# The opening of a fused attention and two-layer kernel: the first two pairs of heads stacked from PSUM instead of by DMA

## The chip, the cores and the metric

The kernel runs on one NeuronCore of a Trainium2 chip. The metric is device time in microseconds (us) of one execution. Engines are named as in the profile: PE is the TensorE matmul engine, DVE is VectorE, ACT is ScalarE, POOL is GpSimd, SP is SyncE (here it only issues DMAs).

## What is computed

```python
# q, k, v: (4, 8, 576, 64) float32; 32 heads in 16 pairs
scores = scale * np.matmul(q, k.transpose(0, 1, 3, 2)); causal mask
a = softmax(scores); local = np.matmul(a, v)
q_p = phi(q)                                  # elu(q) + 1
mem_out = (q_p @ M_prev) / (q_p @ z_prev + 1e-06)
attn = g * mem_out + (1 - g) * local          # g = sigmoid(beta), per head
x = attn as (2304, 512)
x = (s * relu(x @ w_in)**2 + b) @ w_out                # 512 -> 2048 -> 512
out = solu_layernorm(x @ w_in2) @ w_out2               # 512 -> 1024 -> 512
```

## The kernel before

The kernel is three stages one after the other: attention, a squared-relu layer, a second layer. The change touches only how attention begins. Every engine has its own program, written out by hand in order, and the engines meet at semaphores: `sem.wait_ge(n)` holds the whole queue of that engine until the semaphore has reached n. Nothing reorders instructions within an engine.

Attention works on pairs of heads (64 of the 128 partitions each). For each pair `p`:

- SP loads the keys and queries (`load_keys`, `load_queries`) as five tiles of 128 rows; PE turns them (`turn_keys`, `turn_queries`: five 128x128 transposes each) into PSUM.
- To multiply in split precision, each operand is a rounded part and a rest. ACT rounds the keys (`round_keys`) into `cut[p]`, copies the queries into `qT` (`copy_queries`) and once more into `Q1` (`repeat_queries`); POOL rounds the queries (`round_queries`) and takes the rest (`cut_queries`); DVE takes the rest of the keys into `K1` (`cut_keys`).
- The score matmul contracts over 128 partitions: the head's own 64 rows and a second block of 64 rows beside them, kept in `stacked`. Since one of the blocks has to be moved to the other half of the partitions, SP does it with four DMAs from `cut` to `stacked` (`stack(p)`).

For each head `h` PE then makes five tiles of row scores in three steps (`first_rows`, `second_rows`, `third_rows`), each of which waits for the step before to have been read by DVE. DVE takes the row maxima (`row_maximum`, two or more instructions for each step). `first_rows(h+1)` also turns the maxima of head h; DVE copies them (`negT`), POOL spreads them over `Q1` (`spread_maxima`). After that `cross(h, 0..3)` computes the transposed scores minus the maxima, ACT exponentiates them (`exp_weights`), POOL masks the diagonal tiles (`mask_weights`), and `weigh_values(h, ...)` multiplies by the values. `memory(p)` multiplies the features of the queries (`feature_relu`, `feature_exp` on ACT, `features` on POOL) by the memory; DVE scales its result (`scale_memory`).

In the regular steps PE has, in step h, the rows of head h+2, the cross scores of head h and the values of head h-1. The kernel before enters them at h = -6, where most of it is not there yet. The clearing of buffers (memsets) stands at the start of DVE and POOL, and POOL clears `K1` (`clear_keys`) in step -2.

## Time and profile before

| | us |
|---|---|
| median of 3 runs | 879.56 (879.08 to 879.67) |
| profiled execution, time | 879.05 |
| profiled execution, span | 877.3 |
| PE busy | 853.0 (97%) |
| DVE, ACT, POOL busy | 492.0, 312.6, 259.3 |

Time and span of the profiled execution differ by 1.75 us, which lie outside the instructions. PE is busy nearly all the time except in the opening: in the first two of the page's 40 slices it shows 3 and 8 tenths and 9 or more from the third slice to the last but one. A view of the timeline gives each instruction's start and length and, in brackets, how long its engine sat idle before it and what ended that. Busy times of POOL are rough, and the ends of matmuls are modelled.

### The profile page before, as it was taken

How to read it: one execution, taken by the hardware profiler on the slowest of the kernel's cores; microseconds unless marked ns; L12 is line 12 of the kernel's file. 1: busy time of each engine (PE TensorE's matmuls, PEld its weight loads, DVE VectorE, ACT ScalarE, POOL GpSimd, SP SyncE). 2: the span in 40 equal slices, each digit the busy share in tenths (PEclk: the TensorE clock that was granted, in tenths of full speed). 3: DMA queues.
4: the chain of work that ended last, by engine and by line, in shares of the span. 5: the costliest groups of instructions: out<-in, count | busy, mean ns of one | idle time of the engine just before them, and what ended most of it. 6: DMA issues, size and time to landing. Idle time of an engine off the chain costs nothing.

```text
span 877.3 us, 13230 instructions
## 1 busy us (share of the span) xinstructions
PE 853.0 (97%) x4896; PEld 752.0 (86%) x4896; DVE 492.0 (56%) x1025; ACT 312.6 (36%) x564; POOL 259.3 (30%) x369
## 2 busy tenths in 40 slices
PE   3899999999999999999999999999999999999998
PEld 2799999999988888888888889999998888888886
DVE  6566666666546865433443344344758556566664
ACT  3555655656442223222322222232134232223322
POOL 6356565656559994000000000000600000000000
PEclk8799999999999999999999999999999999999999
DMA  7967575756503332000000000000220000000000
GB/s 168 162 141 160 125 155 131 157 129 142 124 1 97 109 107 73 1 1 1 0 1 1 1 0 1 1 1 1 73 72 1 25 25 24 24 24 24 12 24 37
DMA packets 87511, 51.63 MB, mean 59 GB/s; under 512 B 65184, under 2 KB 73376, under 8 KB 87456
## 3 DMA queue, kind: packets, MB, share of 16 engines
q1 hardware_dynamic: 86112, 50.59, 24.1%
q8 instruction: 35, 0.57, 0.3%
q10 hardware_dynamic: 1344, 0.30, 0.2%
q14 instruction: 20, 0.16, 0.1%
HBM read 27.28 MB, written 4.72 MB: 36 GB/s over the span
## 4 chain that ended last, share of the span: by engine, by line
PE 87%; DVE 7%; issue 2%; DMA 1%; POOL 1%; ACT 1%; SPq 0%; ACTq 0%; DVEq 0%; POOLq 0%
PE ps_h L923 7%; PE ps_h L925 7%; PE ps_h L924 7%; PE ps_y L938 7%; PE ps_y L939 7%; PE ps_y L940 7%; PE ps_v L499 7%; PE ps_s L440 4%; PE ps_hid L1199 4%; PE ps_r L1228 4%; PE ps_hid L1201 4%; PE ps_r L1230 4%; PE ps_hid L1200 4%; PE ps_r L1229 4%; PE ps_t L394 2%
## 5 line engine op out<-in xcount | busy, mean ns | idle before, releaser
L1042 DVE TENSOR_TENSOR xT<-xT 128x512 f32<-128x512 f32 (+1 forms) x80 | 60.7, 759 | 134.0 <-ACT xT L998 133.9
L938 PE MATMUL ps_y<-g_hi,wout 128*128 128x512 f32 (+1 forms) x320 | 117.6, 367 | 0.2 <-DVE g_lo L1049 0.2
L923 PE MATMUL ps_h<-x_hi,win 128*128 128x512 f32 (+1 forms) x320 | 117.7, 368 | 0.0
L925 PE MATMUL ps_h<-x_hi,win 128*128 128x512 f32 (+1 forms) x320 | 117.5, 367 | 0.0
L940 PE MATMUL ps_y<-g_hi,wout 128*128 128x512 f32 (+1 forms) x320 | 117.5, 367 | 0.0
L939 PE MATMUL ps_y<-g_lo,wout 128*128 128x512 f32 (+1 forms) x320 | 117.5, 367 | 0.0
L924 PE MATMUL ps_h<-x_lo,win 128*128 128x512 f32 (+1 forms) x320 | 117.5, 367 | 0.0
L499 PE MATMUL ps_v<-v_raw,pT 128*128 128x65 f32 (+1 forms) x960 | 107.5, 254 | 1.2 <-DVE t_loc L740 1.2
L499 PEld LDWEIGHTS ps_v<-v_raw,pT 128*128 128x128 f32 (+1 forms) x960 | 101.2, 173 | 6.6 <-issue 4.5
L678 DVE CUSTOM_DVE_ANT_0 spent<-ps_s,mask 128x576 f32<-128x576 f32 (+4 forms) x160 | 81.6, 539 | 44.4 <-PE ps_s L440 43.7
L561 ACT ACTIVATE pT<-ps_x 128x512 f32<-128x512 f32 (+3 forms) x128 | 64.0, 500 | 99.6 <-PE ps_x L484 98.6
L998 ACT ACTIVATE xT<-ps_h 128x512 f32<-128x512 f32 (+1 forms) x80 | 44.2, 553 | 148.4 <-PE ps_h L925 146.5
L1004 ACT ACTIVATE g_hi<-xT 128x512 fp32r<-128x512 f32 (+1 forms) x80 | 47.2, 590 | 132.3 <-DVE xT L1044 132.3
L1049 DVE TENSOR_TENSOR g_lo<-xT,g_hi 128x512 fp32r<-128x512 f32 (+1 forms) x80 | 63.4, 793 | 51.9 <-ACT g_hi L1004 51.9
L904 POOL TENSOR_SCALAR win<-stage 128x1024 fp32r<-128x1024 f32 x4 | 4.9, 1226 | 280.8 <-PE ps_h L925 280.8
L1186 POOL TENSOR_TENSOR rstd<-variance,minus_half 128x1 f32<-128x1 f32 x18 | 16.8, 931 | 212.8 <-DVE variance L1405 212.8
L344 POOL TENSOR_SCALAR_AFFINE_SELECT pT<-pT 128x128 f32<-128x128 f32 (+1 forms) x160 | 42.4, 284 | 94.9 <-ACT pT L561 94.9
L440 PE MATMUL ps_s<-stacked 128*128 128x512 f32 (+2 forms) x192 | 58.5, 388 | 10.7 <-DMA stacked<-cut 6.2
L938 PEld LDWEIGHTS ps_y<-g_hi,wout 128*128 128x128 f32 x320 | 60.1, 188 | 8.0 <-DVE g_lo L1049 0.5
L925 PEld LDWEIGHTS ps_h<-x_hi,win 128*128 128x128 f32 x320 | 60.1, 188 | 7.6
L923 PEld LDWEIGHTS ps_h<-x_hi,win 128*128 128x128 f32 x320 | 60.1, 188 | 7.5
L924 PEld LDWEIGHTS ps_h<-x_lo,win 128*128 128x128 f32 x320 | 60.1, 188 | 7.5
(130 smaller groups left out, 1677.2 us busy)
## 6 DMA issues: line engine op xcount, KB each, us to landing
stacked<-cut SPq DMA_DIRECT2D x64, 288.0 KB, 5.2
out<-res SPq DMA_DIRECT2D x18, 256.0 KB, 2.0
k_raw<-in_k SPq DMA_DIRECT2D x32, 128.0 KB, 2.6
v_raw<-in_v SPq DMA_DIRECT2D x32, 128.0 KB, 2.7
stage<-in_moe_w_in SPq DMA_DIRECT2D x16, 256.0 KB, 2.7
stage<-in_moe_w_out SPq DMA_DIRECT2D x16, 256.0 KB, 2.6
q_raw<-in_q SPq DMA_DIRECT2D x30, 128.0 KB, 3.7
stage<-in_moe_w_in SPq DMA_DIRECT2D x4, 512.0 KB, 3.4
```

What stands on the lines that cost most here:

```text
L440: ins = pe.matmul(ps_s[:, S_AT[t] + lo:S_AT[t] + hi], stacked[:, a, 0, P * t:P * (t + 1)], stacked[:, a, 1, lo:hi], start=True, stop=True)
L499: ins = pe.matmul(ps_v[0:m, par, E1 * t:E1 * (t + 1)], pT[par][:, at:at + m], v_raw[h // 2 % 3][:, j, par, :], start=(t == 0), stop=(j == ...
L561: act.activation(pT[h % 2][:, chunk_at[c]:chunk_at[c] + chunk_width[c]], ps_x[:, c % 2, 0:chunk_width[c]], ACT.Exp, scale=SCALE).then_inc( ...
L678: return dve.tensor_tensor_reduce(spent[:, at:at + n], ps_s[:, S_AT[t]:S_AT[t] + n], mask[:, FULL * P + r - n:FULL * P + r], -1.0, HUGE, A ...
L923: pe.matmul(out, hi, x_hi[:, k, 0:n], start=(k == 0), stop=False)
L924: pe.matmul(out, hi, x_lo[:, k, 0:n], start=False, stop=False)
L925: ins = pe.matmul(out, lo, x_hi[:, k, 0:n], start=False, stop=(k == KT - 1))
L938: pe.matmul(out, wout[:, f, HI, w], g_hi[:, r, 0:n], start=(f == 0), stop=False)
L939: pe.matmul(out, wout[:, f, HI, w], g_lo[:, r, 0:n], start=False, stop=False)
L940: ins = pe.matmul(out, wout[:, f, LO, w], g_hi[:, r, 0:n], start=False, stop=(f == FT - 1))
L1042: dve.tensor_tensor(r, r, r, ALU.mult).then_inc(square_done, 1)
L1049: dve.tensor_tensor(g_lo[:, f % RING, 0:width(c)], r, g_hi[:, f % RING, 0:width(c)], ALU.subtract)\
```

## The change

The first two pairs (heads 0 to 3) no longer use the DMA to stack. Their tiles are loaded into places with room for three 64-wide blocks (`first_k`, `first_q`, laid over `pT` and `t_mem`); DVE copies the first head's block behind the second's (`double`), so that PE can turn each pair in both head orders (`turn_keys` and `turn_swapped_keys`, and the same for queries). Every block of `stacked` then already lies on the right partitions in PSUM, and ACT (14 instructions named in `BY_ACT`) and DVE (6, in `BY_DVE`) write it from there. POOL repeats head 0's and head 2's queries (`repeat_first`). Pairs from 2 on are stacked by DMA as before. The first two head steps are written out by hand on each engine, in another order; PE starts with ten 128x128 matmuls on the identity (`warm_up`) whose result nobody reads; `memory(1)` moves from step 1 to step 2; the clearing of `K1` on POOL and DVE moves to their opening memsets; the first loads no longer wait for memsets.

```diff
-    t_mem = [sb(f"t_mem{s}", [P, NT, 2, D]) for s in range(3)]
+    all_t_mem = sb("t_mem", [P, 3 * NT * 2 * D])
+    t_mem = [all_t_mem[:, s * NT * 2 * D:(s + 1) * NT * 2 * D].rearrange("p (t two d) -> p t two d", two=2, d=D)
+             for s in range(3)]
...
+    THREE = NT * 3 * D
+    first_k, first_q = ([words_.rearrange("p (t three d) -> p t three d", three=3, d=D) for words_ in places]
+                        for places in ((pT[0][:, 0:THREE], all_t_mem[:, 0:THREE]),
+                                       (pT[1][:, 0:THREE], all_t_mem[:, THREE:2 * THREE])))
...
+    DIRECT = 2
+    BY_ACT = [(0, "k_own0"), (0, "k_moved0"), (0, "q_hi0"), (0, "q_cut0"), (0, "q_hi1"), (0, "q_own1"),
+              (1, "k_moved0"), (1, "k_moved1"), (1, "k_own0"), (1, "q_hi0"), (1, "q_cut0"), (1, "q_hi1"),
+              (1, "k_own1"), (1, "q_own1")]
+    BY_DVE = [(0, "k_own1"), (0, "k_moved1"), (0, "q_lo0"), (0, "q_lo1"), (1, "q_lo0"), (1, "q_lo1")]
+    K_SWAPPED, Q_SWAPPED = (1, 3), (2, 4)
...
+    DVE_CLEARS = PSUM_CLEARS + 3 + 2 * 2
+    WARM = 10
...
-        sp.wait_ge(cleared_dve, 1)
         load_keys(0)
-        sp.wait_ge(cleared_dve, 2)
-        load_queries(0)
-        sp.wait_ge(cleared_dve, 3)
         load_keys(1)
         load_keys(2)
         load_queries(2)
-        stack(0)
-        stack(1)
-        load_keys(3)
         load_memory()
         load_values(0)
+        load_keys(3)
         load_queries(3)
         load_values(1)
-        for h in range(HEADS):
+        stack(2)
+        load_keys(4)
+        for h in range(1, HEADS):
...
-        def clear_keys():
-            pool.memset(words(K1[:, :, :, S:W]), 0.0).then_inc(cleared, 1)
-            pool.memset(words(K1[MINE[0], :, 1, 0:S]), 1.0).then_inc(cleared, 1)
-            pool.wait_ge(cleared, POOL_CLEARS)
+        pool.memset(words(K1[:, :, :, S:W]), 0.0).then_inc(cleared, 1)
+        pool.memset(words(K1[MINE[0], :, 1, 0:S]), 1.0).then_inc(cleared, 1)
+        pool.wait_ge(cleared, POOL_CLEARS)
+        def repeat_first(p):
+            act_placed(pool, p, "q_hi0")
+            pool.tensor_scalar(Q1[MINE[0], p, 0, 0:S], words(stacked[MINE[0], slot(2 * p), 0, 0:S]), 1.0, 1.0,
+                               ALU.mult, ALU.mult).then_inc(repeated, 1)
...
+        repeat_first(0)
+        repeat_first(1)
+        pool.wait_ge(repeated, DIRECT)
+        spread_maxima(0)
+        mask_weights(0, 0)
+        round_queries(2)
+        mask_weights(0, 1)
+        cut_queries(2)
+        features(0)
+        mask_weights(0, 3)
+        features(1)
+        pool.wait_ge(phi_done, 2)
+        spread_maxima(1)
+        mask_weights(1, 0)
+        mask_weights(1, 1)
+        pool.wait_ge(tri_done, NT + 4)
+        spread_maxima(2)
+        mask_weights(1, 3)
...
+        def turn_swapped(raw, into):
+            for t in range(NT):
+                ins = pe.transpose(into[:, P * t:P * (t + 1)],
+                                   raw[:, t, 1:3, :].rearrange("p two d -> p (two d)"), ident[:, :])
+            ins.then_inc(swapped_turned, 1)
+        def warm_up():
+            for _ in range(WARM):
+                pe.matmul(ps_s[:, 0:P], ident[:, :], ident[:, :], start=True, stop=True)
...
+            elif p == 1:
+                act_placed(pe, 0, "k_own0")
+                pe.wait_ge(k_lo_done, 1)
...
+            if h < 2 * DIRECT:
                 p = h // 2
-                pe.wait_ge(stack_landed[p % SLOTS][h % 2], 16 * STACK_DMAS * (p // SLOTS + 1))
+                if h == 0:
+                    act_placed(pe, 0, "q_hi1")
+                    dve_placed(pe, 0, "q_lo0")
...
-                if h == 0:
-                    memory(0)
+                if h == 2:
+                    memory(1)
...
+        warm_up()
+        turn_keys(0)
+        turn_swapped_keys(0)
+        turn_queries(0)
+        turn_swapped_queries(0)
+        turn_swapped_keys(1)
+        first_rows(0)
+        turn_keys(1)
+        second_rows(0)
+        turn_queries(1)
+        third_rows(0)
+        turn_swapped_queries(1)
+        first_rows(1)
+        cross(0, 0)
+        second_rows(1)
+        cross(0, 1)
+        turn_queries(2)
+        third_rows(1)
+        cross(0, 2)
+        cross(0, 3)
+        turn_keys(2)
+        first_rows(2)
+        cross(1, 0)
+        memory(0)
+        weigh_values(0, (0, 1))
+        second_rows(2)
+        cross(1, 1)
+        turn_keys(3)
+        weigh_values(0, (2,))
+        third_rows(2)
+        cross(1, 2)
+        first_rows(3)
+        turn_queries(3)
+        weigh_values(0, (3,))
+        second_rows(3)
+        cross(1, 3)
+        third_rows(3)
+        weigh_values(0, (4,))
...
-        act.wait_ge(cleared_dve, 4)
-        tiles(act, q_raw[1], q, 1, q_in[1])
+        tiles(act, first_q[0], q, 0, q_in[0])
+        tiles(act, first_q[1], q, 1, q_in[1])
...
+        def put(p, what):
+            half, to = int(what[-1]), slot(2 * p + int(what[-1]))
+            if what[:-1] == "k_own":
+                act.wait_ge(kT_turned, p + 1)
+                place, source = stacked[MINE[half], to, 1, 0:S], keys_psum(p)[MINE[half], 0:S]
...
+            act.activation(place, source, ACT.Copy).then_inc(placed_act, 1)
+        for p, what in BY_ACT:
+            put(p, what)
+            if what == "q_own1":
+                copy_queries(p)
+                if p == 0:
+                    open_gates()
+        exp_weights(0, 0)
         feature_relu(0)
+        exp_weights(0, 1)
+        copy_queries(2)
         feature_exp(0)
+        exp_weights(0, 2)
+        feature_relu(1)
+        exp_weights(0, 3)
+        round_keys(2)
+        feature_exp(1)
+        exp_weights(1, 0)
+        repeat_queries(2, 0)
+        exp_weights(1, 1)
+        round_keys(3)
+        repeat_queries(2, 1)
+        exp_weights(1, 2)
+        copy_queries(3)
+        exp_weights(1, 3)
+        feature_relu(2)
+        feature_exp(2)
...
+        dve.memset(words(K1[MINE[1], :, 0, 0:S]), 1.0).then_inc(cleared_dve, 1)
...
+        def double(raw, landed):
+            dve.wait_ge(landed, 16 * Q_DMAS)
+            dve.tensor_copy(raw[:, :, 2, :], raw[:, :, 0, :]).then_inc(doubled, 1)
+        def put_keys():
+            dve.wait_ge(kT_turned, 1)
+            dve.tensor_copy(stacked[MINE[1], slot(1), 1, 0:S], keys_psum(0)[MINE[1], 0:S]).then_inc(placed_dve, 1)
+            dve.wait_ge(swapped_turned, K_SWAPPED[0])
+            dve.tensor_copy(stacked[MINE[0], slot(1), 1, 0:S],
+                            ps_x[:, :, :].rearrange("p two n -> p (two n)")[MINE[0], 0:S]).then_inc(placed_dve, 1)
+        def low_keys(p):
+            act_placed(dve, p, "k_own0")
+            if p == 0:
+                dve_placed(dve, 0, "k_own1")
+            else:
+                act_placed(dve, p, "k_own1")
+            for par in range(2):
+                mine = MINE[par]
+                ins = dve.tensor_tensor(K1[mine, p, par, 0:S], keys_psum(p)[mine, 0:S],
+                                        stacked[mine, slot(2 * p + par), 1, 0:S], ALU.subtract)
+            ins.then_inc(k_lo_done, 1)
...
+        def low_queries(p, par):
+            act_placed(dve, p, ("q_cut0", "q_own1")[par])
+            if par == 1:
+                dve.wait_ge(qT_copied, p + 1)
+            source, high = ((swapped_psum(p), cut[p][MINE[1], Q_HI, :]), (qT[p], Q1[MINE[1], p, 1, 0:S]))[par]
+            dve.tensor_tensor(stacked[MINE[1], slot(2 * p + par), 0, 0:S], source[MINE[1], 0:S], high,
+                              ALU.subtract).then_inc(placed_dve, 1)
...
+        dve.wait_ge(cleared_dve, DVE_CLEARS + 1)
+        double(first_k[0], k_in[0])
+        double(first_q[0], q_in[0])
+        put_keys()
+        double(first_k[1], k_in[1])
+        double(first_q[1], q_in[1])
+        low_keys(0)
+        low_queries(0, 0)
+        low_queries(0, 1)
+        work_out_gates()
+        first_rows(0)
+        second_rows(0)
+        third_rows(0)
+        first_rows(1)
+        low_queries(1, 1)
+        second_rows(1)
+        third_rows(1)
+        first_rows(2)
+        low_keys(1)
+        cut_keys(2)
+        scale_memory(0)
+        second_rows(2)
+        third_rows(2)
+        cut_keys(3)
+        first_rows(3)
+        second_rows(3)
+        third_rows(3)
```

On POOL the opening memsets are followed before by the rounding of the first queries. In these rows `mz` is the memory's buffer, `K` is `K1`, `Q` is `Q1`, and `pT` holds exponentiated scores. Before, from the memset of `mz` to the first spreading of maxima:

```order
L300 MEMSET mz 128x2080
L302 MEMSET Q 64x640 x3
L314 TENSOR_SCALAR cut<-qT 128x576 [waits qT_copied]
L320 TENSOR_TENSOR cut<-qT,cut 128x576 [waits q_hi_done]
L314 TENSOR_SCALAR cut<-qT 128x576 [waits qT_copied]
L320 TENSOR_TENSOR cut<-qT,cut 128x576 [waits q_hi_done]
L305 MEMSET K 128x8x64
L306 MEMSET K 64x4x576
L325 TENSOR_TENSOR fT<-fT,relu_q 128x576 [waits exp_q_done,cleared]
L332 AFFINE_SELECT Q<-negT 5x640 [waits neg_done,phi_done]
```

Now, after the memsets (which now hold both of `K`) and the repeating of head 0's queries, from that of head 2's to the spreading for head 1, the second `Q<-negT`:

```order
L338 TENSOR_SCALAR Q<-stacked 64x576 [waits placed_act]
L363 AFFINE_SELECT Q<-negT 5x640 [waits neg_done,repeated]
L375 AFFINE_SELECT pT<-pT 128x128 [waits exped,neg_spread]
L375 AFFINE_SELECT pT<-pT 128x64
L345 TENSOR_SCALAR cut<-qT 128x576 [waits placed_dve,qT_copied]
L375 AFFINE_SELECT pT<-pT 128x128 [waits exped]
L375 AFFINE_SELECT pT<-pT 128x128
L351 TENSOR_TENSOR cut<-qT,cut 128x576 [waits q_hi_done]
L356 TENSOR_TENSOR fT<-fT,relu_q 128x576 [waits exp_q_done]
L375 AFFINE_SELECT pT<-pT 128x128 [waits exped]
L356 TENSOR_TENSOR fT<-fT,relu_q 128x576 [waits exp_q_done]
L363 AFFINE_SELECT Q<-negT 5x640 [waits neg_done,phi_done]
```

The two memsets of `K` moved ahead of all other work; between the spreading for head 0 and that for head 1 there now stand the rounding and cutting of pair 2 and the features of pairs 0 and 1.

On DVE, before, after the opening memsets:

```order
L707 TENSOR_TENSOR K<-ps_v,cut 64x576 [waits k_hi_done]
L707 TENSOR_TENSOR K<-ps_v,cut 64x576
L758 MEMSET K 64x4x576
L707 TENSOR_TENSOR K<-ps_x,cut 64x576 [waits k_hi_done]
L707 TENSOR_TENSOR K<-ps_x,cut 64x576
L663 TENSOR_SCALAR inv_gate<-beta_in 128x8 [waits gates]
```

Now, at the same place (`pT` and `t_mem` here are the first tiles of pair 0 and pair 1):

```order
L842 MEMSET K 64x4x576
L890 COPY pT<-pT 128x5x64 [waits k_in0,cleared_dve]
L890 COPY pT<-pT 128x5x64 [waits q_in0]
L894 CAST stacked<-ps_v 64x576 [waits kT_turned]
L896 CAST stacked<-ps_x 64x576 [waits swapped_turned]
L890 COPY t_mem<-t_mem 128x5x64 [waits k_in1]
L890 COPY t_mem<-t_mem 128x5x64 [waits q_in1]
L907 TENSOR_TENSOR K<-ps_v,stacked 64x576 [waits placed_dve,placed_act]
L907 TENSOR_TENSOR K<-ps_v,stacked 64x576
L917 TENSOR_TENSOR stacked<-ps_s,cut 64x576 [waits placed_act]
L917 TENSOR_TENSOR stacked<-qT,Q 64x576 [waits qT_copied,placed_act]
```

Four SBUF copies (`double`) and two copies out of PSUM stand ahead of everything that reads the turned tiles.

On PE, before, the first rows of head 2 and the first cross scores of head 0, and what is behind them:

```order
L440 MATMUL ps_s<-stacked 128x512 [waits maxed,stack_landed1_0]
L440 MATMUL ps_s<-stacked 128x64
L440 MATMUL ps_s<-stacked 128x256
L455 MATMUL ps_s<-ident,least 128x128
L483 MATMUL ps_x<-stacked 128x448 [waits neg_spread,cleared_dve,q_again,cleared,k_lo_done]
L484 MATMUL ps_x<-Q,K 128x448
L483 MATMUL ps_x<-stacked 64x64
L484 MATMUL ps_x<-Q,K 64x64
L431 MATMUL ps_t<-mz,fT 128x130 [waits qT_copied,m_in,phi_done]
L431 MATMUL ps_t<-mz,fT 128x130 x4
```

Now the first rows of head 2 stand with the cross scores of head 1, which wait for POOL (`neg_spread`), and the memory product and values are behind them:

```order
L577 MATMUL ps_x<-Q,K 128x320
L439 MATMUL ps_t<-ident,k_raw 128x128 [waits qT_copied,k_in0]
L439 MATMUL ps_t<-ident,k_raw 128x128 x4
L512 MATMUL ps_s<-stacked 128x512 [waits maxed,placed_dve,placed_act]
L512 MATMUL ps_s<-stacked 128x64
L512 MATMUL ps_s<-stacked 128x256
L541 MATMUL ps_s<-ident,least 128x128
L576 MATMUL ps_x<-stacked 128x448 [waits k_lo_done,placed_act,exped,repeated,neg_spread]
L577 MATMUL ps_x<-Q,K 128x448
L576 MATMUL ps_x<-stacked 64x64
L577 MATMUL ps_x<-Q,K 64x64
L503 MATMUL ps_t<-mz,fT 128x130 [waits k_lo_done,qT_copied,m_in,phi_done]
```

The first cross scores of head 0 moved ahead of this place, to behind the first rows of head 1.

## Rows read from the trace of the kernel before

**Rows 1.** The page, section 1 (engine, busy us, share, instructions) and section 5.
```profile
PE 853.0 (97%) x4896; PEld 752.0 (86%) x4896; DVE 492.0 (56%) x1025; ACT 312.6 (36%) x564; POOL 259.3 (30%) x369
...
L499 PE MATMUL ps_v<-v_raw,pT 128*128 128x65 f32 (+1 forms) x960 | 107.5, 254 | 1.2 <-DVE t_loc L740 1.2
```

**Rows 2.** Timeline of PE: start us, us, instruction, [idle before <-releaser].
```profile
6.08 1.30 PE L394 MATMUL ps_v<-ident,k_raw 128*128 128x128 f32 x5 [6.08 <-DMA k_raw<-in_k]
...
17.26 1.19 PE L440 MATMUL ps_s<-stacked 128*128 128x512 f32 x3 [6.18 <-DMA stacked<-cut]
...
28.83 0.72 PE L483 MATMUL ps_x<-stacked 128*128 128x448 f32 x1
...
30.98 2.51 PE L431 MATMUL ps_t<-mz,fT 128*128 128x130 f32 x10 [0.89 <-issue]
...
37.49 0.45 PE L483 MATMUL ps_x<-stacked 128*128 128x448 f32 x1
...
38.37 0.73 PE L394 MATMUL ps_t<-ident,q_raw 128*128 128x128 f32 x5
...
42.74 1.28 PE L431 MATMUL ps_t<-mz,fT 128*128 128x130 f32 x10
...
44.67 0.72 PE L440 MATMUL ps_s<-stacked 128*128 128x512 f32 x3
...
45.26 0.46 PE L483 MATMUL ps_x<-stacked 128*128 128x448 f32 x1
```

**Rows 3.** Windows of PE: stretch, length, busy (instructions), granted clock, DMA share, GB/s.
```profile
13.00:14.00 1.00, 0.00 (x0) 1.00 0.62 131
14.00:15.00 1.00, 0.00 (x0) 0.62 0.91 187
...
34.00:35.00 1.00, 0.87 (x5) 0.64 0.54 121
```

**Rows 4.** Timeline of POOL, same columns.
```profile
5.53 1.77 POOL L302 MEMSET Q<- 64x640 f32 x3
...
14.04 0.54 POOL L305 MEMSET K<- 128x512 f32 x1
14.50 2.01 POOL L306 MEMSET K<- 64x2304 f32 x1
16.59 1.40 POOL L325 TENSOR_TENSOR fT<-fT,relu_q 128x576 f32<-128x576 f32 x1
24.69 0.74 POOL L332 TENSOR_SCALAR_AFFINE_SELECT Q<-negT 5x640 fp32r<-5x640 f32 x1 [6.70 <-DVE negT L687]
30.85 0.48 POOL L344 TENSOR_SCALAR_AFFINE_SELECT pT<-pT 128x128 f32<-128x128 f32 x2 [5.42 <-ACT pT L561]
...
32.22 0.67 POOL L314 TENSOR_SCALAR cut<-qT 128x576 fp32r<-128x576 f32 x1
```

**Rows 5.** Timeline of DVE, same columns.
```profile
13.62 2.92 DVE L663 TENSOR_SCALAR inv_gate<-beta_in 128x8 f32<-128x8 f32 x1
...
16.81 1.21 DVE L667 TENSOR_SCALAR inv_rest<-inv_rest 128x8 f32<-128x8 f32 x1
```

**Rows 6.** DVE groups by form: shapes xcount | busy us, mean ns | idle before.
```profile
L678 DVE CUSTOM_DVE_ANT_0 spent<-ps_s,mask 128x576 f32<-128x576 f32 x32 | 23.9, 747 | 0.7 <-DVE inv_rest L671 0.2
...
L678 DVE CUSTOM_DVE_ANT_0 spent<-ps_s,mask 128x512 f32<-128x512 f32 x32 | 22.1, 691 | 14.5 <-PE ps_s L440 14.5
...
L707 DVE TENSOR_TENSOR K<-ps_t,cut 64x576 fp32r<-64x576 f32 x28 | 21.1, 753 | 0.2
...
L724 DVE TENSOR_TENSOR t_mem<-ps_t,rm 128x640 f32<-128x640 f32 x16 | 13.2, 824 | 0.5
...
L687 DVE COPY negT<-ps_s 5x128 f32<-5x128 f32 x32 | 9.1, 283 | 5.2 <-PE ps_s L455 4.7
```

**Rows 7.** Timeline of ACT, same columns.
```profile
30.12 0.60 ACT L561 ACTIVATE pT<-ps_x 128x512 f32<-128x512 f32 x1 [2.02 <-PE ps_x L484]
```

**Rows 8.** DMA issues of 12 to 21 us: xcount, KB each, median us to landing.
```profile
stacked<-cut SPq DMA_DIRECT2D x8, 288.0 KB, 5.2
```

164 lines of the change are left out of this document (108 added, 56 removed).

## The prediction

> **What bounds the kernel now.** I read the page first: PE is busy 853.0 of 877.3 us, 97% [rows 1]. So nothing counts but what makes PE wait, and the page's slices put that in the opening. The timeline of PE shows where: PE sat idle for 6.18 us before the first score matmul at 17.26, waiting for the DMA that stacks [rows 2]. From 44.67, the first rows of head 4, the three kinds of PE work of a head step follow each other without a gap [rows 2], and the program from there on is the same before and after but for one step that moves behind it. So 44.67 is my landmark: the change is worth what it moves that point, less what it pushes behind it. The windows show a second cost. The granted clock falls within 14.00 to 15.00, about 3 us after PE's last work (17.26 less 6.18 is 11.08), to 0.50, which is 1.2 of 2.4 GHz, and comes back only within 34.00 to 35.00 [rows 3]. At half clock the memory product takes 2.51 us, at full clock 1.28; the first rows take 1.19 and 0.72 [rows 2].
>
> **What is taken out.** Pairs 0 and 1 no longer wait for eight stacking DMAs, 5.2 us from issue to landing each [rows 8]. The 6.18 us wait at 17.26 goes. PE also gets ten matmuls on the identity from about 1.5 us, when the identity exists; five of 130 columns took 2.51 at half clock [rows 2], so ten of 128 take some 5, and they end about when the first keys land, near 6 [rows 2]. They delay nothing and leave the clock high or about to rise. I cost them at nothing; if they overran the keys by 1 us, that would still lie inside the next wait.
>
> **The first new wait: DVE's copies behind POOL's memsets.** PE can turn the swapped keys only after DVE has copied a block from SBUF to SBUF (`double`). No such copy is in the trace. The nearest row is DVE's `TENSOR_SCALAR` of 8 elements from SBUF to SBUF at 13.62: it took 2.92 us, to 16.54, while POOL worked through a tensor operation and the two memsets of `K`, which end at 16.51; the one at 16.81 took 1.21, until POOL's 1.40 from 16.59 ended [rows 4, 5]. So such an instruction does not get in between POOL's instructions, not even between memsets. POOL's memsets of `Q` end at 7.30 and the two of `K`, 0.54 and 2.01 long, now stand right behind them [rows 4], to 9.8. I let both first copies wait until 9.8, at 0.3 us each (320 columns; bounds: nothing, and the 0.69 of a 512-wide read [rows 6]). The other bound is no wait, a start near 6.1.
>
> The Trainium skill, SBUF — State Buffer, section "Who interferes with whom", says that a DVE copy that runs in a mode with both ports and any GpSimd instruction exclude each other, and VectorE: DVE Perf Modes, section "Mode 2×_2P", gives the shapes for it, which 5 by 64 to 5 by 64 in float32 meets. By that rule the copies wait as the two rows did, so it gives the same 9.8; the trace agrees for the scalar form only.
>
> **From there to the first cross scores, DVE's queue sets the time.** From 9.8: two copies 0.6; two copies from PSUM 1.4 (576 wide, 0.75 each, 0.70 from start to start); two more copies 0.6; the rests of the keys 1.5; those of the queries 1.5; the gates 1.0. That is 16.4. PE's first rows of head 0 are done before that (it needs the last of the swapped queries, near 12, then three ACT writes of 0.6 each and one rest, about 14.7). Then the maxima, which in three steps read 832, 512 and 512 columns (1.05, 0.7 and 0.7 by the rows of 576 and 512 columns), with a PE step of about 0.3 beyond the overlap between each: 19.4. First rows of head 1 0.8, `negT` 0.3, the rest of a query 0.75: cross scores of head 0 at **21.4** [rows 2, 6]. Before, they began at 28.83, so 7.4 us are won here.
>
> **The second new wait: the cross scores of head 1 behind POOL's new order.** They need the spread maxima of head 1, which POOL now does after the features of pair 0 and 1. From 21.4: cross 0.76, exponential 0.60 for 512 columns [rows 7], and by its size two relus of 576 at 0.6 from start to start, a second exponential 0.5 and the copy of queries 2 0.65: 25.1. Then POOL: rounding 0.67, masks 0.5, cutting 1.4, features 1.4, mask 0.3, features 1.4, spreading 0.74, together 6.4 [rows 4]: cross scores of head 1 at **31.6**. All that PE has until then (rows of head 1 and 2, the rest of head 0's cross scores, two turns of 0.6) ends near 26.4. So PE idles for 5.2 us. Queued behind are the memory product, the values of head 0 and the second rows of head 2. Before, the cross scores of head 1 began at 37.49 [rows 2], so 5.9 of the 7.4 us are left.
>
> **To the landmark.** From 31.6: cross 0.6, memory 1.28, DVE's scaling 1.2 (0.82 for its last instruction, two small ones ahead), the turn of keys 3 (waits for it) 0.6, values 0.7 (a value matmul is 107.5/960, or 0.11 [rows 1], and there are six), third rows of head 2: 36.6. DVE: maxima 0.7, rests of keys 3 1.5, `negT` and first maxima of head 3 1.4: 40.2. PE by then: turn of queries 3 (waits for the rests), eight value matmuls, second rows: 40.85; DVE 0.7, third rows, 0.75: **42.5** at full clock [rows 2, 6].
>
> **The clock.** An idle time of 5.2 us is nearly as long as the one of 6.18 before, in which the clock fell after about 3 us [rows 2, 3]. So I take it that it falls again, and comes back only after PE has been busy some microseconds. On the chain after 31.6 there are then cross 0.6 and memory 1.28 at double length: 1.9 us more. Bounds: nothing (no fall) and 2.8 (rows of head 2 and the turn too). I take 1.9: **44.4**.
>
> **Moved behind the landmark:** `memory(1)`, 1.28 us, 1.2 from start to start, all on PE, which is the bound there. The stacks of pair 2 are issued from about 28, when the queries are cut, and at 5.2 each [rows 8] they land some 7 us before the landmark, so head 4 does not wait for them.
>
> **Sum.** 44.4 + 1.2 - 44.7 = 0.9 us later. Against the profiled execution's 879.05 that is 879.95; its time lies 0.5 below the median of the three runs, so for the median I take half of that on top: **880.1**. What a measurement of this kernel can tell from no change is about 0.2%, 1.8 us. So the likeliest result is no change that can be measured: some 6 us won up to head 1 are given back to a PE that waits for POOL, runs at half clock and has a product left to do.
>
> **Rivals.**
>
> *The clock holds (chance 0.17).* The 5.2 us wait lets it stand, since the warm matmuls and a shorter wait shift its time. For it: one fall in one trace is little to go by. Against: 5.2 us is well past the 3 after which it fell. Time 880.1 - 1.9 = 878.2.
>
> *The copies do not wait for POOL (0.12).* DVE starts at 6.1 instead of 9.8; of the 3.7 us, 2.5 reach the end, since the turns of pair 1 then wait for their own loads, which are issued behind those of pair 0. Time 877.6. Against it are the two rows at 13.62 and 16.81; for it, that they are of another instruction.
>
> *The chain through POOL and DVE is shorter than I sum (0.10).* Spans on POOL are rough; if its seven instructions take 1 us less, the idle time is 4 us, the clock may stand, and the hand-offs that I priced at a full step overlap. 1.9 + 1.5 less: 876.7.
>
> *Slower (0.23): the clock also falls in the first wait.* PE has nothing from 7.2, when the first keys are turned, to 10.1. That is 2.9 us; before, it fell about 3 us after the last work, so 0.3 us decide. It then stays low as it did from 17 to 34, where PE waited again and again for about as long as the 0.89 at 30.98 [rows 2]. Price: the turns and rows between the maxima of head 0 and 1 doubled, 2 us; the first rows and cross of head 1 and 0, 0.7; and the two steps after 31.6 already counted, with the rows and the values before the landmark, 1 more. Time 880.1 + 3.7 = 883.8; with a part of it 882.
>
> The rest (0.38) is my forecast, with its own range of 878.8 to 881.8.
>
> **How the numbers follow.** Of the forecast's 0.38 I put 0.31 within 0.2% of 879.56 and 0.07 above; of the first rival 0.13 within and 0.04 below; of the second 0.09 below and 0.03 within; the third's 0.10 below; of the fourth 0.20 above and 0.03 within. That is faster 0.23, same 0.50, slower 0.27. The range for 8 in 10 leaves out one tenth on either side: it begins at the third rival's 876.5 and ends at 883.2, inside the fourth.
>
> **What the profile after would show.** Right: DVE's first copy starting (or ending) at about 9.8 and not 6; first score rows near 14.7; cross scores of head 0 near 21.4 and of head 1 near 31.6, with a PE idle time of some 5 us released by POOL; a granted clock of 0.50 behind it; the first rows of head 4 near 44, and the same spacing from there but for the memory product. Wrong: the copy ending at 6.4; no fall of the clock; the cross scores of head 1 more than 2 us from 31.6, which would make one of the sums above wrong; or a change of time that lies behind the landmark.

## The result, and the profile after

The changed kernel ran at a median of 880.78 us over 20 runs (880.10 to 881.90, one at 885.43), the kernel before at 879.71 (879.03 to 880.14, 20 runs). The ratio is 1.0018 with a 95% interval of 1.0011 to 1.0025. So the change makes the kernel slower by 0.1 to 0.25%, 1 to 2 us, which lies inside the 0.2% (1.8 us) that I had called the least that can be told from no change; with 20 runs each, the interval is only 0.07% to either side. The forecast was 880.1, no measurable change, with 0.9 us later as its sum.

The 20 times fall in two groups: eleven from 880.10 to 880.93 and eight from 881.62 to 881.90, with one apart at 885.43. The profiled execution took 880.93, with a span of 879.2.

The timeline of PE after the change shows the places that the forecast named. Columns are as in [rows 2].

```profile
1.58 4.64 PE L453 MATMUL ps_s<-ident 128*128 128x128 f32 x20 [1.58 <-POOL ident L314]
6.01 1.19 PE L439 MATMUL ps_v<-ident,pT 128*128 128x128 f32 x5
...
10.28 0.76 PE L447 MATMUL ps_x<-ident,t_mem 128*128 128x128 f32 x5 [1.44 <-DVE t_mem L890]
13.24 0.70 PE L512 MATMUL ps_s<-stacked 128*128 128x512 f32 x3 [2.19 <-DVE stacked L917]
...
17.90 1.27 PE L447 MATMUL ps_x<-ident,t_mem 128*128 128x128 f32 x5
...
22.14 0.44 PE L576 MATMUL ps_x<-stacked 128*128 128x448 f32 x1 [1.67 <-ACT Q L757]
...
32.11 0.74 PE L576 MATMUL ps_x<-stacked 128*128 128x448 f32 x1 [5.01 <-POOL Q L363]
...
33.20 2.52 PE L503 MATMUL ps_t<-mz,fT 128*128 128x130 f32 x10
...
45.44 0.70 PE L512 MATMUL ps_s<-stacked 128*128 128x512 f32 x3 [0.27 <-DVE least L861]
...
46.58 1.36 PE L503 MATMUL ps_t<-mz,fT 128*128 128x130 f32 x10
```

The line at 10.28 is the swapped keys of pair 1, the one at 17.90 its swapped queries, the two at 32.11 and 33.20 the cross scores of head 1 and the memory product. The wait of 6.18 us at 17.26 [rows 2] is gone, the first score rows start at 13.24, and the first cross scores at 22.14 instead of 28.83. Then PE idles for 5.01 us until POOL has spread the maxima of head 1, the memory product behind that takes 2.52 us, and the first rows of head 4 start at 45.44, 0.77 us later than before.

The windows of PE (columns as in [rows 3]) show two falls of the granted clock, within 13 to 14 and at the end of 30 to 31, and the second return within 37 to 38.

```profile
13.00:14.00 1.00, 0.76 (x5) 0.91 1.20 124
14.00:15.00 1.00, 0.99 (x5) 0.50 1.32 157
20.00:21.00 1.00, 0.47 (x2) 0.67 0.82 183
30.00:31.00 1.00, 0.00 (x0) 0.95 0.89 180
37.00:38.00 1.00, 1.00 (x6) 0.64 0.22 46
```

On DVE the four copies look like this (timeline of DVE; the group `x2` is two instructions).

```profile
5.86 1.22 DVE L890 COPY pT<-pT 128x320 f32<-128x320 f32 x2 [0.35 <-DMA pT<-in_k]
...
8.71 2.28 DVE L890 COPY t_mem<-t_mem 128x320 f32<-128x320 f32 x2
```

And on POOL (timeline of POOL), its memsets of `Q` and `K` beside them, and the chain in front of the cross scores of head 1.

```profile
5.53 2.05 POOL L330 MEMSET Q<- 64x640 f32 x3
7.54 0.52 POOL L332 MEMSET K<- 128x512 f32 x1
8.00 2.01 POOL L333 MEMSET K<- 64x2304 f32 x1
10.10 0.67 POOL L338 TENSOR_SCALAR Q<-stacked 64x576 fp32r<-64x576 f32 x1
...
25.74 0.67 POOL L345 TENSOR_SCALAR cut<-qT 128x576 fp32r<-128x576 f32 x1 [1.62 <-ACT qT L707]
...
31.32 0.74 POOL L363 TENSOR_SCALAR_AFFINE_SELECT Q<-negT 5x640 fp32r<-5x640 f32 x1
```

The copies of pair 0 got in between POOL's memsets of `Q` (which took 2.05 us together instead of 1.77 [rows 4]). Of those of pair 1, the first took 1.52 us, to 10.23, past the end of POOL's long memset at 10.01, and the second 0.84, to 10.99, past the end of POOL's next instruction at 10.77.

**An account that closes.** The landmark is the start of the first rows of head 4. If it carries everything, span less landmark must be the same for all kernels with the same program behind it. Before it is 877.3 - 44.67 = 832.6. After it is 879.2 - 45.44 = 833.8: 1.1 us more, which is the memory product that moved behind it (1.36 long at 46.58, PE being busy there). So of the 1.9 us by which the two spans differ, 0.8 is the landmark and 1.1 the moved product.

### The profile page after: what moved, and what is told of

It reads as the page before. It is cut to its first block, busy times and chain, and to the rows that moved or that the text cites. A ratio compares the mean times of both kernels' runs of the same rounds, so it can differ in the third digit from the quotient of the medians.

```text
span 879.2 us, 13335 instructions
## 1 busy us (share of the span) xinstructions
PE 857.4 (98%) x4936; PEld 757.1 (86%) x4936; DVE 495.5 (56%) x1038; ACT 317.5 (36%) x572; POOL 256.9 (29%) x367
## 4 chain that ended last, share of the span: by engine, by line
PE 86%; DVE 7%; issue 2%; POOL 1%; ACT 1%; ACTq 0%; POOLq 0%
PE ps_h L1165 7%; PE ps_h L1166 7%; PE ps_h L1167 7%; PE ps_y L1180 7%; PE ps_y L1181 7%; PE ps_y L1182 7%; PE ps_v L595 7%; PE ps_hid L1441 4%; PE ps_r L1470 4%; PE ps_hid L1443 4%; PE ps_r L1472 4%; PE ps_hid L1442 4%; PE ps_r L1471 4%; PE ps_s L512 3%; PE ps_t L503 2%
## 5 line engine op out<-in xcount | busy, mean ns | idle before, releaser
L861 DVE CUSTOM_DVE_ANT_0 spent<-ps_s,mask 128x576 f32<-128x576 f32 (+4 forms) x160 | 81.6, 539 | 44.4 <-PE ps_s L512 43.8
L576 PE MATMUL ps_x<-stacked 128*128 128x448 f32 (+2 forms) x192 | 60.1, 321 | 7.1 <-POOL Q L363 5.0
L1165 PEld LDWEIGHTS ps_h<-x_hi,win 128*128 128x128 f32 x320 | 60.0, 188 | 7.6
L1181 PEld LDWEIGHTS ps_y<-g_lo,wout 128*128 128x128 f32 x320 | 60.1, 188 | 7.5
```

Of the source, the lines that this page charges most:

```text
L576: pe.matmul(out, stacked[:, a, 1, some], stacked[:, a, 0, lo:hi], start=True, stop=False)
L861: return dve.tensor_tensor_reduce(spent[:, at:at + n], ps_s[:, S_AT[t]:S_AT[t] + n], mask[:, FULL * P + r - n:FULL * P + r], -1.0, HUGE, A ...
L1165: pe.matmul(out, hi, x_hi[:, k, 0:n], start=(k == 0), stop=False)
L1181: pe.matmul(out, wout[:, f, HI, w], g_lo[:, r, 0:n], start=False, stop=False)
```

## Experiments

Each ran beside the kernel before on the same chip, 9 to 12 times (e10 five times), and each ratio is to the kernel before there. The kernel before had a median of 879.19 beside e1, e2, e4 and e5, of 879.41 beside e6 to e9 and of 879.66 beside e10 to e13, so medians of different groups can differ by up to 0.5 us for that reason alone; the ratio is taken over all runs and is not the quotient of the two medians. "Landmark" is read from the one profiled execution, which is not always a typical one: in e1 and e13 it was the fastest of all, in e5 and e7 the slowest. The mean granted clock of the last two columns (1 is 2.4 GHz, 0.5 is 1.2) is read from windows over 11 to 27 and 27 to 49 us.

| kernel | median us (range) | ratio, 95% interval | landmark | span - landmark | clock 11:27 | 27:49 |
|---|---|---|---|---|---|---|
| before | 879.71 (879.03 to 880.14) | 1 | 44.67 | 832.6 | 0.60 | 0.82 |
| changed | 880.78 (880.10 to 885.43) | 1.0018, 1.0011 to 1.0025 | 45.44 | 833.8 | 0.79 | 0.84 |
| e1, POOL's order | 880.27 (879.11 to 882.88) | 1.0019, 1.0009 to 1.0029 | 43.59 | 833.8 | 0.68 | 0.92 |
| e2, wait filled | 878.53 (878.17 to 879.76) | 0.9992, 0.9983 to 1.0001 | 43.01 | 833.7 | 0.68 | 1.00 |
| e4, K1 cleared later | 880.43 (878.86 to 882.54) | 1.0010, 1.0001 to 1.0019 | 46.69 | 833.8 | 0.63 | 0.81 |
| e5, before filled | 880.04 (878.93 to 882.32) | 1.0005, 0.9997 to 1.0014 | 47.10 | 833.5 | 0.83 | 0.74 |
| e6, copies undisturbed | 879.39 (878.92 to 881.45) | 1.0005, 0.9997 to 1.0014 | 43.50 | 833.8 | 0.68 | 0.84 |
| e7, POOL's order and DVE's | 881.03 (876.31 to 883.66) | 1.0000, 0.9984 to 1.0017 | 47.56 | 834.3 | 0.61 | 0.66 |
| e8, e6 and e7 | 879.71 (873.65 to 881.78) | 0.9994, 0.9978 to 1.0011 | 43.84 | 833.8 | 0.68 | 0.77 |
| e9, e2 and e6 | 878.46 (876.03 to 880.74) | 0.9984, 0.9975 to 0.9993 | 41.95 | 833.8 | 0.68 | 1.00 |
| e10, e8 filled | 876.92 (874.78 to 877.46) | 0.9960, 0.9947 to 0.9974 | 41.47 | 833.8 | 0.58 | 0.99 |
| e11, no warm-up | 880.53 (880.12 to 884.25) | 1.0019, 1.0010 to 1.0029 | 44.60 | 833.8 | 0.68 | 0.84 |
| e12, product back | 880.03 (879.74 to 881.33) | 1.0006, 0.9997 to 1.0015 | 45.59 | 832.8 | 0.68 | 0.84 |
| e13, before, load early | 878.01 (877.67 to 878.24) | 0.9983, 0.9974 to 0.9992 | 43.30 | 832.7 | 0.61 | 0.90 |

The column "span - landmark" is the account again: 832.6 to 832.8 with the product ahead of the landmark, 833.7 to 833.8 with it behind. Two do not fit: e7, whose clock came back only after the landmark (below), and e5, with 0.9 us more than before. Its trace has that 0.9 far behind the opening: it is 2.39 us behind the kernel before at 272 us and 3.29 at 279, and between them stands a wait of 0.45 us for POOL (`win`, the weights of the second stage) that the kernel before does not have.

### The wait for POOL, taken away or filled

e1 puts the spreading of head 1's maxima ahead of two operations that PE does not need yet:

```diff
         mask_weights(0, 1)
-        cut_queries(2)
         features(0)
+        pool.wait_ge(phi_done, 1)
+        spread_maxima(1)
+        cut_queries(2)
         mask_weights(0, 3)
         features(1)
-        pool.wait_ge(phi_done, 2)
-        spread_maxima(1)
```

> One part undone: on POOL the spreading of head 1's maxima stands behind the features of pair 0 and ahead of the cutting of pair 2's queries and the features of pair 1, so it can end near 29 instead of 32.06. Theory A (PE's wait for POOL ahead of the cross scores of head 1, and the clock that falls in it, ate the gain): cross scores of head 1 near 29.1; the memory product then waits for DVE's rests of pair 2's keys, which end at 31.4, so the landmark (first rows of head 4, now 45.44) comes 1.8 us earlier if the clock still falls and 3.0 if it holds, 879.0 or 877.8 us. Theory B (the wait is idle time that costs nothing, since DVE's queue sets the landmark): the cross scores move and the landmark does not, 880.8. Theory C (the cost is only in the first fall of the clock at 13.8): 880.8 as well.

e2 leaves the wait and fills it with idle work:

```diff
+        def keep_busy(n, out):
+            for _ in range(n):
+                pe.matmul(out, ident[:, :], ident[:, :], start=True, stop=True)
...
         first_rows(2)
+        pe.wait_ge(exped, 3)
+        keep_busy(20, ps_x[:, 0, 0:P])
         cross(1, 0)
```

> The changed kernel with 20 more matmuls of 128x128 on the identity in PE's wait ahead of the cross scores of head 1 (from 27.1, about 4.4 us at full clock), results read by nobody. The wait stays, the idle time goes. Theory A: the clock holds through the wait; cross scores of head 1 still at 32.1, the memory product takes 1.3 us instead of 2.5, the landmark comes 1.8 to 2.3 us earlier, about 878.8 us, and the spread of the changed kernel's times (880.1 to 881.9) narrows. Theory B: granted clock 1.00 there, landmark within 0.3 us of 45.44, 880.8.

The timeline of PE in e1 shows two waits of 1.91 us in place of one of 5.01.

```profile
29.20 0.47 PE L576 MATMUL ps_x<-stacked 128*128 128x448 f32 x1 [1.91 <-POOL Q L363]
...
31.87 2.22 PE L503 MATMUL ps_t<-mz,fT 128*128 128x130 f32 x10 [1.91 <-DVE K L925]
```

The landmark came 1.85 us earlier and the profiled time was 879.11, as theory A had it with a falling clock. But that execution was the fastest of nine. The median, 880.27, is only 0.5 below the changed kernel's, and the ratio, 1.0019, is the same; theory A's 879.0 lies outside its interval. By its times alone, e1 speaks for theory B. In e2 the cross scores of head 1 started at 32.05, as late as before the edit, and yet the landmark came 2.43 us earlier. The timeline of PE and two windows show why: the clock, which was at half until 27.0 in this execution, stays up from there, and the memory product takes 1.36 us.

```profile
27.55 4.63 PE L457 MATMUL ps_x<-ident 128*128 128x128 f32 x40
32.05 0.47 PE L580 MATMUL ps_x<-stacked 128*128 128x448 f32 x1
...
32.65 1.36 PE L507 MATMUL ps_t<-mz,fT 128*128 128x130 f32 x10
```

```profile
26.00:27.00 1.00, 1.00 (x7) 0.50 0.09 25
32.00:33.00 1.00, 1.00 (x9) 1.00 0.91 184
```

Its median is 2.25 us below the changed kernel's (0.9992 against 1.0018 in ratio), its times span 1.6 us, and the group near 881.7 is gone. Theory B falls: with the wait as long as ever and only the clock kept up, the landmark moves. What the wait costs by its length is not told by these two runs, since e1 shortened it with the clock still falling.

### DVE's copies and POOL's memsets

e4 clears `K1` after the repeating of head 0's queries; e6 does the same, but also holds POOL until all four copies are made. The first added line is in e6 alone:

```diff
-        pool.memset(words(K1[:, :, :, S:W]), 0.0).then_inc(cleared, 1)
-        pool.memset(words(K1[MINE[0], :, 1, 0:S]), 1.0).then_inc(cleared, 1)
-        pool.wait_ge(cleared, POOL_CLEARS)
+        pool.wait_ge(doubled, 2 * DIRECT)
+        pool.wait_ge(cleared, POOL_CLEARS - 2)
...
         repeat_first(0)
+        pool.memset(words(K1[:, :, :, S:W]), 0.0).then_inc(cleared, 1)
+        pool.memset(words(K1[MINE[0], :, 1, 0:S]), 1.0).then_inc(cleared, 1)
+        pool.wait_ge(cleared, POOL_CLEARS)
```

> One part undone: POOL's two memsets of K1 (0.52 and 2.01 us) stand behind the repeating of head 0's queries instead of ahead of it. Theory A: DVE's copies of pair 1 at 8.71 no longer wait and take about 0.7 us instead of 2.28, so the first score rows start near 11.6 instead of 13.24, and 1.6 us reach the landmark, 879.2; if PE's shorter idle time also keeps the clock, 1 to 2 us more, 877.7. Theory C (the first fall of the clock matters more than the copies): the granted clock stays 1.00 at 14 us and the time is under 878. Rival: the cross scores of head 0 are held by the loads and turns of pair 1, so nothing moves behind 22 us, 880.8.

> As the changed kernel, but POOL waits after its memsets of Q1 until DVE has made all four copies, repeats head 0's queries, and only then clears K1. The last experiment moved the clearing and put it right on the copies; here nothing of POOL lies on them. Theory A: the copies of pair 1 take 0.36 us each, the first score rows start near 11.7 instead of 13.24, and about 1.2 us reach the first cross scores and the landmark: 879.6, and 1 to 2 us less if the clock stays up in the shorter wait. Rival: the cross scores of head 0 are held by ACT's writes of pair 1, which follow PE's turns, and the gain ends there: 880.8.

e4 missed: the first score rows came at 14.38, later than the 13.24 of the changed kernel and not at 11.6, and the time was 880.43 where 879.2 was expected. But it showed the mechanism better than a hit. The two copies of pair 1 in e4 (one line's instructions on DVE: min/median/max in ns), and POOL's timeline beside them:

```profile
L891 DVE COPY t_mem<-t_mem x2: 359/1809/3259, 8.6 to 8.9; 128x320 f32<-128x320 f32 x2
```

```profile
8.83 0.67 POOL L336 TENSOR_SCALAR Q<-stacked 64x576 fp32r<-64x576 f32 x1 [1.24 <-ACT stacked L758]
9.45 0.52 POOL L407 MEMSET K<- 128x512 f32 x1
9.90 2.01 POOL L408 MEMSET K<- 64x2304 f32 x1
```

The first copy, with POOL idle, took 0.359 us. The second was issued at 8.9, just after POOL's first instruction, and took 3.259 us, past the end of all three. In e6, with nothing of POOL on them, the same view has

```profile
L892 DVE COPY t_mem<-t_mem x2: 347/353/359, 8.7 to 9.0; 128x320 f32<-128x320 f32 x2
```

and the first score rows started at 11.58 instead of 13.24, the first cross scores at 20.46 instead of 22.14. So the copies' wait was worth 1.7 us there. The median is 879.39, 1.4 us below the changed kernel's, where theory A had 879.6; by the ratios, 1.0005 against 1.0018, it is 1.1 us, and the two intervals overlap a little.

### Both, and the clock

e7 is e1 with DVE's two pairs of rests exchanged, since the second wait of e1 was for the later one (the counts that PE waits for are changed to match); e8 adds e6; e9 is e2 with e6; e10 is e8 with both waits filled.

```diff
         first_rows(2)
-        low_keys(1)
         cut_keys(2)
+        low_keys(1)
         scale_memory(0)
```

```diff
         first_rows(2)
+        pe.wait_ge(exped, 3)
+        keep_busy(7, ps_x[:, 0, 0:P])
         cross(1, 0)
+        pe.wait_ge(exped, 4)
+        keep_busy(5, ps_x[:, 1, 0:P])
         memory(0)
```

> The POOL order of the first experiment, and DVE takes the rest of pair 2's keys ahead of that of pair 1's, so that the memory product, which needs their PSUM, can start 1.5 us earlier. In the first experiment PE waited twice, 1.91 us for POOL and 1.91 us for DVE. Theory A: cross scores of head 1 near 29.2 again, memory product near 30.2 instead of 31.87, PE's idle time there under 2.5 us together; landmark near 42 against 43.59 and 45.44, 877.5 us if the clock stays up, 879 if it falls. Theory B (DVE's queue sets the landmark, and this only swaps two of its instructions): as the first experiment, 880.3.

> Both: POOL's order and DVE's swap as in e7, and POOL clear of the copies as in e6. If the two waits are in series, their gains add: landmark near 41 and 876.5 us, faster than both kernels. If the clock's fall decides instead, the time scatters by the 1.5 us that a fall costs and the median stays near 878.

> The changed kernel with 20 idle matmuls in PE's wait for POOL (as in the second experiment, which took 2.25 us off the changed kernel's median) and POOL clear of the copies (as in e6). The filled wait keeps the clock up behind it; what e6 gains comes on top: 877.3 us, landmark near 41.8. If the copies do not matter, as the second experiment, 878.5.

> The combination of POOL's order, DVE's swap and the undisturbed copies, with PE's two waits there filled: 7 identity matmuls ahead of the cross scores of head 1 (1.36 us of waiting) and 5 ahead of the memory product (0.91 us), results read by nobody. Unfilled, this combination ran from 873.65 to 881.78 us. Theory A' (what is left of the scatter is the clock falling after about 28 us, into waits that are short): the clock stays up from about 27 on, all runs between 873.5 and 877, median near 875.5, landmark near 40. Rival: the fall is decided by the waits ahead of 23 us, which are not filled; then it scatters as before and the median stays at 878 to 880.

e7, e8 and e9 all missed. e7 ran from 876.31 to 883.66 us and e8 from 873.65 to 881.78: the executions of one program lie up to 8 us apart, where I had expected scatter of 1.5 us at most, and the medians are 881.03 and 879.71 instead of 877.5 and 876.5. Five of e7's twelve times lie between 876.31 and 877.94, where the sum of its steps puts it, the rest above 880.9. e9 has its landmark at 41.95, as forecast, but its median, 878.46, is that of e2 again and not 877.3, so its times do not show that the gain of e6 comes on top; two of its twelve times hold 3.4 and 3.7 us outside the span instead of the usual 1.7.

Each run's mean granted clock over its whole span is also measured, and in these kernels the time follows it. In e8 it is 0.998 at 873.65 us, 0.992 at 876.53 and 876.62, 0.988 at 879.39 and 879.71, and 0.984 at 881.78; in e7 it goes from 0.994 at 876.31 to 0.984 at 883.66. The groups of the changed kernel differ in the same way: 0.990 to 0.992 in the eleven, 0.988 in the eight, 0.985 at 885.43. It does not hold everywhere: a run of e11 took 884.25 at 0.992, and runs of the kernel before that show 1.0 are mostly no faster than those at 0.988, which is not explained here. At the same clock of 0.998, the fastest runs of e8 and e9 took 873.65 and 876.03, so the shorter waits of e8 seem worth some 2.4 us where the clock does not fall; that is one run against one.

The profiled execution of e7 was 883.66, and its windows show the clock going down three times, the last one within 41 to 42 and back only within 48 to 49:

```profile
14.00:15.00 1.00, 0.50 (x5) 0.79 1.12 168
28.00:29.00 1.00, 1.00 (x7) 0.89 0.00 0
31.00:32.00 1.00, 0.06 (x2) 0.82 0.00 0
38.00:39.00 1.00, 1.00 (x10) 0.77 0.94 168
41.00:42.00 1.00, 0.38 (x3) 0.94 0.85 192
48.00:49.00 1.00, 1.00 (x6) 0.65 0.00 0
```

PE's idle times there were 1.25, 1.19, 0.70 and 0.62 us, each with work behind it. The two waits that e10 fills are these in the timeline of PE in e8:

```profile
27.46 0.47 PE L578 MATMUL ps_x<-stacked 128*128 128x448 f32 x1 [1.36 <-POOL Q L362]
...
29.13 2.50 PE L505 MATMUL ps_t<-mz,fT 128*128 128x130 f32 x10 [0.91 <-DVE K L927]
```

In e10 the same stretches as above, with two of these waits filled:

```profile
13.00:14.00 1.00, 0.00 (x0) 0.82 1.04 87
27.00:28.00 1.00, 1.00 (x9) 0.85 0.06 16
31.00:32.00 1.00, 1.00 (x11) 1.00 0.00 0
38.00:39.00 1.00, 0.97 (x9) 1.00 0.94 193
41.00:42.00 1.00, 0.74 (x7) 1.00 0.66 152
48.00:49.00 1.00, 1.00 (x13) 1.00 0.00 0
```

Its five times lie within 2.7 us, and it beats both kernels: 0.9960 of the kernel before, 0.9947 to 0.9974, clear of e8's 0.9978 to 1.0011, which is the same program without the filling. The rival had the time scatter as before with a median of 878 to 880, and it did not, so the waits behind 27 us decided most of it. Not all of it went, and five runs say little about what is left: the median is 1.4 us more than expected, the landmark 41.47 instead of 40, and the spans of e9, filled in one place only, still range over 3.1 us.

### The parts that I had costed at nothing or from one row

```diff
-        warm_up()
         turn_keys(0)
```

> One part undone: without the ten matmuls ahead of the first turns. I costed them at nothing. The first turns then run at half clock, 1.1 us from start to start instead of 0.55, and the swapped queries of pair 0 are turned about 1.1 us later; ACT's writes are 0.65 each behind them, so the first score rows come at most 1 us later, 14.2. Theory A: the landmark moves by at most that 1 us and the clock's later falls decide the rest, 880.8 to 881.8. Rival (the warm matmuls are what makes the clock fall at 13.8, since it rises too early to last): first fall later or none, time under 880.

Without the warm-up the first score rows start at 13.24, exactly as with it, and the ratio is that of the changed kernel. Costing it at nothing was right. The swapped keys of pair 1 wait for DVE's copies either way, 1.44 us with the warm-up and 0.61 without, so those copies hide it; it was not tried without it in a kernel with undisturbed copies.

e12 moves the product back, on PE behind `third_rows(3)`:

```diff
-                if h == 2:
-                    memory(1)
...
         third_rows(3)
+        memory(1)
         weigh_values(0, (4,))
```

`scale_memory(1)` goes back to the end of DVE's step 1 in the same way. (This is an edit of the changed kernel, as are all but e5 and e13.)

> One part undone: the memory product of pair 1 stands again in step 1, between the third rows of head 3 and the last values of head 0, instead of in step 2; DVE's scaling of it goes with it. From the trace: behind the landmark it cost 1.13 us (from the first rows of head 4 to the end, 833.76 against 832.63). Ahead of it PE has 0.27 us of waiting left to put it in. Theory A: landmark 0.9 later, the rest 1.13 shorter, 880.6. Rival: DVE's scaling ahead of the maxima of head 4 makes more waiting, 881.3.

The median is 880.03, 0.75 us below the changed kernel's where I expected 0.2, and 1.1 us by the ratios (1.0006 against 1.0018); the two intervals overlap. I had the landmark 0.9 us later for the product ahead of it, and it came only 0.15 later, at 45.59. The account is clear: span less landmark is back at 832.8.

### What the kernel before hid

e5 fills the 6.18 us wait of the kernel before, ahead of the first score rows:

```diff
                 ahead, here, behind = is_head(h + 2), is_head(h), is_head(h - 1)
+                if h == -2:
+                    for _ in range(26):
+                        pe.matmul(ps_s[:, 0:P], ident[:, :], ident[:, :], start=True, stop=True)
                 if ahead or is_head(h + 1):
```

> The kernel before with 26 matmuls of 128x128 on the identity between the last turn of queries (11.07) and the first score rows (17.26), results read by nobody; nothing else changed. It asks what the clock alone was worth before. If the clock holds from then on, my sum of the steps between 17.3 and the landmark at full clock gives first rows of head 4 about 1.3 to 2 us earlier, 877.9 to 878.4. Rival: the chain there is DVE's and POOL's, and PE's half clock is hidden: 879.7.

That did not help: 880.04, a ratio of 1.0005 (0.9997 to 1.0014). It did not keep the clock up for long either: in the profiled execution, the slowest of the eleven, the clock held through the filled wait, fell within 21 to 22 and was back only within 38 to 39. So the question what the clock alone was worth before is not answered. The timeline of PE in e5 says what stood behind the filled wait.

```profile
32.60 2.51 PE L431 MATMUL ps_t<-mz,fT 128*128 128x130 f32 x10 [3.39 <-issue]
```

The cross scores before it came 0.87 us earlier than before, and then the memory product waited 3.39 us for no instruction of any engine; in the kernel before it is 0.89, also put down to "issue" [rows 2]. The last load of the memory was issued at 27.9 in e5 and at 26.0 before, and the product started 4.7 and 5.0 us later, which is what these loads take from issue to landing (4.4 to 5.8). e13 loads the memory earlier in the kernel before:

```diff
         stack(1)
-        load_keys(3)
         load_memory()
+        load_keys(3)
```

> The kernel before with only one thing changed: SP loads the memory ahead of the keys of pair 3 instead of behind them. In the trace of before, PE sat idle 0.89 us ahead of the memory product for no reason that the profile shows, and in the filled kernel before 3.39 us; both end about 4.9 us after the last of those loads was issued. If that is the load's landing, it now comes near 28, the idle time ahead of the product is gone, and the landmark comes up to 0.9 us earlier, 878.7. If it is something else, 879.5 as before.

It ran at 878.01, within 0.6 us in all eleven runs, 0.9983 of the kernel before (0.9974 to 0.9992): the product started at 30.06 with no wait ahead of it, and the landmark came 1.37 us earlier, more than the 0.9 expected, since the clock also came back sooner (0.90 instead of 0.82 from 27 to 49). So "issue" there was a landing DMA, and a move of one line makes the kernel before 0.17% faster, while the whole change made it 0.18% slower.

## Why the prediction held, point by point

**What bounds the kernel, and the landmark.** Right: the landmark and the moved product account for the spans of twelve of the fourteen kernels within 0.2 us.

**The first new wait.** Half right. The mechanism, a copy that waits for POOL, is shown: 0.36 us alone, 3.26 behind three instructions of POOL. The time of 9.8 was wrong: the copies of pair 0 got in at 5.86, between the memsets of `Q`, and ended at 7.08; only those of pair 1 were held, to 10.99. So the step that failed is "such an instruction does not get in between POOL's instructions, not even between memsets". It did between those of `Q`, it did not between those of `K`, and why is open. "The copy starting or ending at about 9.8" was a sign of being right, and it fits only the first copy of pair 1, which ended at 10.23. The Trainium skill, SBUF — State Buffer, section "Who interferes with whom", has the pair of ports held for a whole instruction by whichever issues first; the copies of 0.36 us and of 3.26 us agree that it is exclusive, but three instructions in a row went ahead of one copy in e4, which is more than one instruction's turn.

**To the first cross scores.** I summed DVE's queue to 21.4; they came at 22.14. That is luck in part, since two errors cancel. DVE took its first maxima at 14.88, 1.5 us earlier than the 16.4 of the sum, but then waited for PE (0.54, 0.90 and 1.59 us) and ended its last rest at 21.58. What released the cross scores was ACT, writing pair 1 behind PE's last swapped turn, and PE made those turns at half clock (1.21 to 1.27 us each), since the clock fell at 13.8. The forecast had no fall here. I had this fall as the rival "slower", at 2.9 us of idling; it happened in waits of 1.44 and 2.19 us. So the mechanism of that rival is what ran, and the forecast's time held because its price of 3.7 us was too high: the clock was back within 20 to 21, not after the landmark.

**The second wait.** Right in place and size: cross scores of head 1 at 32.11 (31.6), 5.01 us of idling (5.2), released by POOL's spreading. POOL's instructions from 25.74 to 32.06 (eight of them; the text on the third rival says seven) are 6.3 us (6.4).

**The clock.** It fell, as forecast. I took 1.9 us and bounded it by 2.8; e2 measured 2.4 at the landmark and 2.25 at the median, so the term was 0.3 to 0.5 too small.

**Moved behind the landmark.** 1.2 forecast, 1.1 found.

**The sum** came to 0.9; the two profiled executions differ by 1.9 and the medians by 1.07. The landmark was forecast at 44.4 and came at 45.44. The direction was right, and the forecast was 0.7 us short of the median. (Two small slips of adding do not matter: 879.95 and half of 0.5 make 880.2 and not 880.1, and the third rival's time is 876.7 where it is worked out and 876.5 in the range.) What I did not see at all is that each number for the clock is one draw out of several: the median of a kernel with such waits is not the time of one trace. The changed kernel's own trace has two falls; those of e1, e4, e6, e8, e11 and e12 have three or four, one of them between 21 and 24 us.

**The stacks of pair 2 and the warm-up**, costed at nothing, cost nothing.

So where did the gain go? The change wins 6.7 us at the first cross scores (22.14 against 28.83) and 5.4 at those of head 1 (32.11 against 37.49). From there to the landmark it needs 13.33 us where the kernel before needs 7.18, and that takes all of it back: the memory product and the second and third rows of head 2, which before stood ahead of the cross scores of head 1, now stand behind PE's wait for POOL, and 2.4 us of the difference is the clock that falls in this wait (e2). Behind the landmark the moved product costs 1.1 more (e12 takes it back). The wait for POOL itself was 5.01 us, of which e1 removed 3.1, with 1.9 of that coming back as a wait for DVE's rests. The copies held by POOL's memsets cost 1.1 to 1.4 (e6), which the 6.7 already contain. These numbers are not terms of one sum.

## What to carry to other kernels

Find the instruction from which the program runs without gaps, and keep the account of what lies behind it: here it closed within 0.2 us for twelve of fourteen kernels. When an opening is reordered, look at every other engine's queue for work that nobody needs yet in front of something that PE waits for; keeping POOL's memsets off DVE's copies, moving two POOL operations back and two DVE operations around, and filling what was left of the waits, turned 1.0018 into 0.9960. Rank edits by many runs and not by one trace. A kernel whose times scatter by several us between runs may be at a clock that falls in some and not in others: compare the granted clock over the same stretch before believing one trace.

## What the runs showed of the hardware

- The clock fell in waits much shorter than I thought necessary. I had 3 us from the one fall before; it fell within 41 to 42 in e7 behind idle times of 0.70 and 0.62 us, and in the changed kernel behind 1.44 and 2.19. In e6 it fell within 21 to 22 with PE at work since 20.46, behind a wait of 1.67. Filling two waits of 1.36 and 0.91 us (e8) with twelve matmuls (e10) kept it at 0.99 on average from 27 to 49 us, against 0.77, in the two profiled executions.
- Where it falls moves from run to run of one program. e1 and e2 are the same program up to about 26 us and ran on one chip, but their profiles show the first fall within 11 to 12 and within 13 to 14. e8 and e10 are the same up to the first wait that e10 fills, near 27 us, but show the clock at a mean of 0.68 and 0.58 from 11 to 27 (on two chips). The Trainium skill, TensorE: Matmul & The Clock Gate, section "What's actually happening", says that the gate's measuring runs freely and does not start with the kernel. The traces agree with it, in that the first fall moves as just said and that e8's times range over 8 us; that this is the cause is not shown.
- A float32 copy of 320 columns from SBUF to SBUF takes DVE 0.36 us alone and up to 3.26 beside POOL.
- A wait that the profile puts down to "issue" was a DMA's landing: 0.89 us in the kernel before, gone in e13, where the load was issued earlier.
